# Strassen products of an MLP: operand sums made one product earlier, first summands written into accumulating banks

## The chip, the core and the metric

The kernel runs on one core of a Trainium2 chip. The time is the device time of one execution, in microseconds (us). Five engines work side by side, each with its own list of instructions: PE (TensorE, matmuls), ACT (ScalarE), DVE (VectorE), POOL (GpSimd) and SP (SyncE, which here issues all DMAs). They wait for each other by semaphores: `wait_ge(s, v)` holds an engine until the semaphore s has reached v.

## The reference

Batch 8, sequence 576, model width 512, all in fp32. An attention-like stage and a first mixing stage come first; the change is in the last stage:

```
def _moe2_ref(x, w_tok1, w_tok2, w_ch1, w_ch2):
    xt = x.transpose(0, 2, 1)
    h = np.maximum(xt @ w_tok1, 0.0) @ w_tok2
    u = x + h.transpose(0, 2, 1)
    h2 = np.maximum(u @ w_ch1, 0.0) @ w_ch2
    return (u + h2).astype(np.float32)
```

u has 8*576 = 4608 rows (tokens) of 512; `w_ch1` is 512 x 1536 and `w_ch2` is 1536 x 512. The output is [8, 576, 512].

## The kernel before, in words

Four phases follow each other: A (attention and first mixing), B (token mixing, which makes u), C (the **first product**, g = relu(u w_ch1)) and D (the **second product**, out = u + g w_ch2). Phases hand each other work at the seams through `nxt` and `prev`.

Each fp32 matmul is made of three: the operand is split into a rounded part `hi` (a copy to fp32r by ACT) and a rest `lo` (a subtraction by DVE), and `split_matmul` does hi*hi, hi*lo and lo*hi. C and D also use the Strassen-Winograd form: a 2x2 block product with seven block products (FIRST, SECOND, SHARED, MIDDLE, THIRD, LATE, LAST) in place of eight. The price is sums: four sums of the weight's blocks (made once), four sums of the moving operand's blocks per group, and seven sums of the results.

The tokens come in six **groups** of 768. C does 36 **units** (six groups of NI = 6 slices of w_ch1's columns); a unit is seven products of two depth tiles, 42 matmuls of 128x384. Its operand is `raw_u`, loaded once a group; `prep_hi` and `prep_lo` (L1222, L1226) split it, POOL makes its four sums (`prep_sum`). Results leave a bank by ACT copies (L1380, L1385, L1392) and DVE additions; a relu of all four blocks (L1366) ends the unit, and SP stores the blocks in `g_scratch` (L1316). Beside it, every second unit takes one of 14 steps that split `w_ch2` and its sums (ACT L1282, POOL L1292, stores L1273 and L1274).

D does six groups; a group is seven products for two column tiles j with six depth tiles, 252 matmuls of 128x384. SP loads the four blocks of g (`raw_g`, L1496). Two of the four operand sums are made by POOL (`first_sum`, `third_sum`: L1764, L1770), two by DVE (L1717, L1722). Each product needs a split: ACT L1528, DVE L1532. Its seven result sums, and the additions of u (`u2_left`), are shared by ACT, DVE and POOL (L1773, L1778); DVE transposes each result (L1679), and SP stores it in four DMAs of 48 KB (L1544). The seven split weights (`weights_down`, 1536 KB each) are read at the seam of C and D, as the memory of C's weights comes free.

The order of the work is written out by hand: each engine's list is the order of the calls in `scalar`, `vector`, `gpsimd`, `tensor` and `sync`. All DMAs go through SP's one queue.

## Time and profile before

| | us |
|---|---|
| median of 3 runs | 1306.64 (1303.24 to 1309.28) |
| the profiled execution, whole | 1305.25 |
| its span, first to last instruction | 1303.4 |
| phases A and B, until the last matmul before C | 0 to 708 |
| C, first product | 708 to 981 |
| D, second product | 981 to 1303.4 |

Busy shares of the span are 93% for PE, 60% DVE, 43% POOL, 39% ACT. A busy share averages phases with different limits, so the table is to be read by phase. PE's busy time contains the overlap of neighbouring matmuls: what counts for the time is the distance between their starts, and the idle time in front of them.

### The profile page before, as it was taken

How to read it: one execution, taken by the hardware profiler on the slowest of the kernel's cores; microseconds unless marked ns; L12 is line 12 of the kernel's file. 1: busy time of each engine (PE TensorE's matmuls, PEld its weight loads, DVE VectorE, ACT ScalarE, POOL GpSimd, SP SyncE). 2: the span in 40 equal slices, each digit the busy share in tenths (PEclk: the TensorE clock that was granted, in tenths of full speed). 3: DMA queues.
4: the chain of work that ended last, by engine and by line, in shares of the span. 5: the costliest groups of instructions: out<-in, count | busy, mean ns of one | idle time of the engine just before them, and what ended most of it. 6: DMA issues, size and time to landing. Idle time of an engine off the chain costs nothing.

```text
span 1303.4 us, 20411 instructions
## 1 busy us (share of the span) xinstructions
PE 1215.8 (93%) x7746; PEld 1175.6 (90%) x7746; DVE 787.4 (60%) x1120; ACT 503.3 (39%) x747; POOL 565.6 (43%) x331
## 2 busy tenths in 40 slices
PE   6899999999999999899999999999994599999998
PEld 5799999999999989799899899899994599899997
DVE  3866667665757666655455445444422688777865
ACT  3534333332424242423333455545541334324331
POOL 4443535253434444402631444544410574485473
PEclk9999999999999999999999999999997799999999
DMA  9921424242424200325464555555349276476462
GB/s 253 172 46 43 77 67 72 72 72 72 72 72 72 45 27 0 116 90 180 159 204 152 191 203 229 198 194 209 155 184 404 95 204 193 95 224 183 120 189 49
DMA packets 249438, 177.82 MB, mean 136 GB/s; under 512 B 196256, under 2 KB 221472, under 8 KB 247456
## 3 DMA queue, kind: packets, MB, share of 16 engines
q1 hardware_dynamic: 249376, 176.98, 46.3%
q8 instruction: 41, 0.67, 0.2%
q14 instruction: 21, 0.17, 0.0%
HBM read 109.31 MB, written 67.63 MB: 136 GB/s over the span
## 4 chain that ended last, share of the span: by engine, by line
PE 49%; issue 15%; DVE 13%; POOL 10%; DMA 6%; ACT 4%; SPq 3%; DVEq 0%; POOLq 0%; ACTq 0%
PE bank L42 13%; PE bank L43 12%; PE bank L44 12%; DVE z_g_split L1532 3%; PE bank L1163 2%; PE bank L1165 2%; PE bank L1164 2%; POOL tokens_raw_g L1764 2%; PE bank L236 2%; DMA u_raw_g<-g_scratch 2%; DVE weights_fraction L605 1%; PE bank L918 1%; POOL z_z L770 1%; POOL weights_down_t L1778 1%; DMA tokens_raw_g<-g_scratch 1%
## 5 line engine op out<-in xcount | busy, mean ns | idle before, releaser
L42 PE MATMUL bank<-weights_tok,z_z 128*128 128x288 f32 x576 | 175.1, 304 | 14.7 <-ACT z_z L455 9.3
L43 PE MATMUL bank<-weights_tok,z_z 128*128 128x288 f32 x576 | 171.0, 297 | 0.0
L44 PE MATMUL bank<-weights_tok,z_z 128*128 128x288 f32 x576 | 170.9, 297 | 0.0
L770 POOL TENSOR_TENSOR z_z<-tokens_cos,z_z 128x512 fp32r<-128x512 f32 x32 | 51.8, 1618 | 177.3 <-ACT z_z L455 176.4
L42 PEld LDWEIGHTS bank<-weights_tok,z_z 128*128 128x128 f32 x576 | 109.4, 190 | 18.2 <-ACT z_z L455 10.7
L755 POOL TENSOR_TENSOR weights_rms_inverse<-weights_mean_squares,weights_minus_half 128x8 f32<-128x8 f32 x40 | 65.6, 1640 | 137.7 <-DVE weights_mean_squares L572 137.5
L42 PE MATMUL bank<-z_g_split,weights_down 128*128 128x384 f32 x240 | 83.7, 349 | 36.8 <-DVE z_g_split L1532 36.8
L43 PEld LDWEIGHTS bank<-weights_tok,z_z 128*128 128x128 f32 x576 | 109.5, 190 | 0.0
L44 PEld LDWEIGHTS bank<-weights_tok,z_z 128*128 128x128 f32 x576 | 109.3, 190 | 0.0
L1532 DVE TENSOR_TENSOR z_g_split<-tokens_raw_g,z_g_split 128x2304 fp32r<-128x2304 f32 x16 | 65.2, 4074 | 45.0 <-ACT z_g_split L1528 45.0
L462 ACT ACTIVATE weights_x_channel_major<-u_u 128x288 fp32r<-128x288 f32 x64 | 28.4, 444 | 150.2 <-DVE u_u L633 150.2
L43 PE MATMUL bank<-z_g_split,weights_down 128*128 128x384 f32 x240 | 83.0, 346 | 0.0
L44 PE MATMUL bank<-z_g_split,weights_down 128*128 128x384 f32 x240 | 82.8, 345 | 0.0
L42 PEld LDWEIGHTS bank<-z_g_split,weights_down 128*128 128x128 f32 x240 | 47.2, 197 | 38.2 <-issue 38.2
L42 PE MATMUL bank<-weights_x_channel_major,weights_ch 128*128 128x288 f32 x256 | 77.5, 303 | 0.0
L43 PE MATMUL bank<-weights_x_channel_major,weights_ch 128*128 128x288 f32 x256 | 75.4, 294 | 0.0
L44 PE MATMUL bank<-weights_x_channel_major,weights_ch 128*128 128x288 f32 x256 | 75.4, 294 | 0.0
L1528 ACT ACTIVATE z_g_split<-tokens_raw_g 128x2304 fp32r<-128x2304 f32 x16 | 34.1, 2129 | 100.8 <-POOL tokens_raw_g L1764 43.2
L44 PE MATMUL bank<-z_u_slot,weights_up 128*128 128x384 f32 x216 | 72.2, 334 | 0.0
L42 PE MATMUL bank<-z_u_slot,weights_up 128*128 128x384 f32 x216 | 72.2, 334 | 0.0
L43 PE MATMUL bank<-z_u_slot,weights_up 128*128 128x384 f32 x216 | 72.1, 334 | 0.0
L631 DVE TENSOR_TENSOR u_u<-bank,weights_x_channel_major 128x288 f32<-128x288 f32 x64 | 29.1, 455 | 68.3 <-PE bank L44 67.6
(234 smaller groups left out, 3767.0 us busy)
## 6 DMA issues: line engine op xcount, KB each, us to landing
g_scratch<-attention_staged SPq DMA_DIRECT2D x36, 768.0 KB, 3.3
tokens_raw_g<-g_scratch SPq DMA_DIRECT2D x12, 1152.0 KB, 7.4
weights_down<-w_scratch SPq DMA_DIRECT2D x7, 1536.0 KB, 13.6
x_scratch<-u_u SPq DMA_DIRECT2D x8, 1152.0 KB, 4.2
u_scratch<-u_u SPq DMA_DIRECT2D x8, 1152.0 KB, 6.3
weights_raw_u<-u_scratch SPq DMA_DIRECT2D x6, 1536.0 KB, 9.1
qkv_u_left<-u_scratch SPq DMA_DIRECT2D x6, 1536.0 KB, 6.6
qkv_k<-in_k_dram SPq DMA_DIRECT2D x32, 256.0 KB, 4.7
```

The costliest lines, as they stand in the source:

```text
L42: eng.matmul(out, w[0], x[0], start=first, stop=False)
L43: eng.matmul(out, w[0], x[1], start=False, stop=False)
L44: return eng.matmul(out, w[1], x[0], start=False, stop=last)
L236: mm = pe.matmul(ps_out[j % 2][:, hp * P:(hp + 1) * P], qt[:, j % 2, hp, :], kvbd[:, hp, :], start=True, stop=True)
L462: act.activation(x_half(0, c, half), u[:, c, half * HALF:(half + 1) * HALF], ACT.Copy).then_inc(a_uhi, 1)
L631: dve.tensor_tensor(ug, ps_acc[g % 4][:, 0:HALF], x_half(0, c, half).bitcast(F32), ALU.add).then_inc(d_u1, 1)
L755: gp.tensor_tensor(rms_inv[:, i, :], msq[:, i, :], minus_half[:, :], ALU.pow).then_inc(g_pow, 1)
L770: gp.tensor_tensor(z[1][:, j, :], cos_t[:, j % 3, :], z[0][:, j, :].bitcast(F32), ALU.subtract).then_inc(g_zlo, 1)
L1163: eng.matmul(out, w[0], x[0], start=False, stop=False, skip_group_check=True)
L1164: eng.matmul(out, w[0], x[1], start=False, stop=False, skip_group_check=True)
L1528: act.activation(slot(g, k)[0][:, :, :], operand(g, k)[:, :, :], ACT.Copy).then_inc(a_hi, 1)
L1532: dve.tensor_tensor(slot(g, k)[1][:, :, :], operand(g, k)[:, :, :], slot(g, k)[0][:, :, :].bitcast(F32), ALU.subtract).then_inc(d_lo, 1)
```

## The change

**Operand sums.** C makes not only the four blocks of g but also the four sums that D needs, and stores seven blocks of 128x384 per unit (`g_scratch` grows from 4 to NP = 7 blocks). D loads seven ready operands a group into a ring of four buffers (`load_operand`), splits each and makes no sums. The order of the products is now FIRST, SHARED, MIDDLE, SECOND, THIRD, LATE, LAST.

**First summands.** Where a result was bank + tile in SBUF, the first summand is now written into the bank itself (ACT copies bank to bank, L1402 and L1418 of the new file; DVE adds into a bank) and the product accumulates onto it. Four short matmuls (`open_bank`) open these banks at C's start. In D, DVE writes u + summand into the bank.

**C's order.** Three of a unit's products (THIRD, LATE, LAST) run inside the next unit, between its own four. ACT does each block's relu on its own as it leaves the bank, DVE makes the sums t1 to t4 in `staged`. The store of unit n is issued two units later. Three of a group's splits (`PREP_OWN`) are made in the group's own first unit, four (`PREP_NEXT`) in units 2 to 5 of the group before; `raw_u` is loaded in unit 1 and not in unit 0.

**POOL.** It has nothing left in D, and in C no result sums.

**The seam.** D's weights 1 to 6 are read in two parts around the store of unit 34; the third operand waits for that store, the fourth for the last one. D's first product for j = 0 runs before C's last.

```diff
--- before.py
+++ after.py
...
-    PREP_LO = {(B - 3, 4): 0, (B - 3, 5): 1, (B - 2, 4): 2, (B - 1, 2): 3}
+    PREP_HI = {B - 3: [FIRST], B - 2: [SHARED], B - 1: [MIDDLE, SECOND]}
+    PREP_LO = {(B - 3, 4): FIRST, (B - 2, 4): SHARED, (B - 1, 2): MIDDLE, (B - 1, 4): SECOND}
...
+FIRST, SHARED, MIDDLE, SECOND, THIRD, LATE, LAST = range(NP)
...
+    def bank(i):
+        return banks[i][:, 0:CH]
+    def bank_a(n):
+        return bank(n % 2)
+    def bank_b(n):
+        return bank(2 + n % 2)
+    bank_c, bank_e, bank_f = bank(4), bank(5), bank(6)
...
-    PREP_LO = {(1, 1): [FIRST], (2, 1): [SECOND], (3, 1): [SHARED], (4, 1): [MIDDLE], (5, 0): [THIRD],
-               (5, 1): [LATE], (5, 2): [LAST]}
-    PREP_SUM = {1: [0], 2: [1], 3: [2], 4: [3]}
...
+    PREP_NEXT = {2: [FIRST], 3: [SHARED], 4: [MIDDLE], 5: [SECOND]}
+    PREP_OWN = [THIRD, LATE, LAST]
+    PREP_SUM = {2: [0], 3: [1, 2], 5: [3]}
...
+    def store(sp, n):
+        g, i = divmod(n, NI)
+        sp.wait_ge(d_t4, n + 1)
+        sp.dma_start(g_dram[g, :, i, :, :], staged[n % 2][:, :, :]).then_inc(s_g[n % 2], DMA)
...
-            if i == 0 and g + 1 < NG:
+            if i == 1 and g + 1 < NG:
                 load(sp, g + 1)
             if n == 2 * NP + 1:
                 w2_load(sp, 1)
...
-            sp.wait_ge(a_relu, n + 1)
-            sp.dma_start(g_dram[g, :, i, :, :], staged[n % 2][:, :, :]).then_inc(s_g[n % 2], DMA)
+            if n >= 2:
+                store(sp, n - 2)
             if n in W2_UNIT:
                 w2_store(sp, W2_UNIT[n])
...
+            if n == UNITS - NI + 2:
+                sp.wait_ge(p[LAST], n - 2)
...
                 nxt["load_first"](sp)
+        nxt["load_weights"](sp, range(1, 5))
+        store(sp, UNITS - 2)
+        nxt["load_weights"](sp, range(5, NP))
+        sp.wait_ge(s_g[0], DMA * UNITS // 2)
+        nxt["load_third"](sp)
+        store(sp, UNITS - 1)
...
+        def open_bank(out):
+            pe.matmul(out, wu[FIRST][0][:, 0, 0:P], slot(0, FIRST)[0][:, 0, :], start=True, stop=True)
...
+        for n in range(UNITS):
+            wait(pe, d_c22, n - 1)
+            wait(pe, a_f, n - 1)
+            if n == 0:
+                pe.wait_ge(a_hi, 1)
+                for b in (bank_b(0), bank_b(1), bank_c):
+                    open_bank(b)
+                pe.wait_ge(*prev["d_u"])
+                open_bank(bank_f)
+            product(n, FIRST, bank_a(n))
+            if n > 0:
+                third(n - 1)
+            wait(pe, a_t5, n)
+            product(n, SHARED, bank_e)
+            if n > 0:
+                late(n - 1)
+            pe.wait_ge(a_b, n + 1)
+            product(n, MIDDLE, bank_a(n), onto=True)
+            product(n, SECOND, bank_b(n), onto=True)
+            if n > 0:
+                last(n - 1)
+        third(UNITS - 1)
+        late(UNITS - 1)
+        nxt["first"](pe, 0, 0)
+        last(UNITS - 1)
...
+        def relu(n, k, src, ready, done):
+            act.wait_ge(*ready)
+            act.activation(staged[n % 2][:, k, :], src, ACT.Relu).then_inc(done, 1)
+        def relu21(n):
+            relu(n, SECOND, bank_f, (p[LAST], n + 1), a_g21)
+        for n in range(UNITS + 2):
+            if n >= 2:
+                relu21(n - 2)
+            if n < UNITS:
+                if n == 0:
+                    act.wait_ge(*prev["d_u"])
+                act.wait_ge(p[FIRST], n + 1)
+                act.activation(bank_b(n), bank_a(n), ACT.Copy).then_inc(a_b, 1)
+            if 1 <= n <= UNITS:
+                if n == 2:
+                    act.wait_ge(*prev["stored"])
+                wait(act, s_g[(n - 1) % 2], DMA * ((n - 1) // 2))
+                relu(n - 1, FIRST, bank_b(n - 1), (p[SECOND], n), a_g11)
+                relu(n - 1, LATE, bank_c, (p[THIRD], n), a_g12)
+            if n < UNITS:
+                act.wait_ge(p[SHARED], n + 1)
+                wait(act, d_c22, n - 1)
+                act.activation(t5[n % 2][:, :], bank_e, ACT.Copy).then_inc(a_t5, 1)
+            if n == UNITS:
+                nxt["hi"](act, 0, SHARED)
+            if 1 <= n <= UNITS:
+                act.wait_ge(p[LATE], n)
+                wait(act, a_g21, n - 1)
+                act.activation(bank_f, bank_a(n - 1), ACT.Copy).then_inc(a_f, 1)
+                relu(n - 1, THIRD, staged[(n - 1) % 2][:, THIRD, :], (d_c22, n), a_g22)
+            if n < UNITS:
+                g, i = divmod(n, NI)
+                if i == 0:
+                    for k in PREP_OWN:
+                        prep_hi(act, g, k)
+                elif g + 1 < NG:
+                    for k in PREP_NEXT.get(i, []):
+                        prep_hi(act, g + 1, k)
+                if n in W2_UNIT:
+                    w2_hi_step(act, W2_UNIT[n])
...
+        def t4(n):
+            st = staged[n % 2]
+            dve.wait_ge(a_g21, n + 1)
+            dve.wait_ge(d_t2, n + 1)
+            dve.tensor_tensor(st[:, LAST, :], st[:, SECOND, :], st[:, MIDDLE, :], ALU.subtract).then_inc(d_t4, 1)
+        def t1(n):
+            st = staged[n % 2]
+            dve.wait_ge(a_g11, n + 1)
+            dve.wait_ge(a_g12, n + 1)
+            dve.tensor_tensor(st[:, SHARED, :], st[:, LATE, :], st[:, FIRST, :], ALU.subtract).then_inc(d_t1, 1)
+        def c22(n):
+            dve.wait_ge(a_f, n + 1)
+            wait(dve, s_g[n % 2], DMA * (n // 2))
+            dve.tensor_tensor(staged[n % 2][:, THIRD, :], bank_a(n), t5[n % 2][:, :], ALU.add).then_inc(d_c22, 1)
+        def u4(n):
+            dve.wait_ge(p[MIDDLE], n + 1)
             dve.wait_ge(a_t5, n + 1)
...
+            wait(dve, a_g12, n)
+            dve.tensor_tensor(bank_c, bank_a(n), t5[n % 2][:, :], ALU.add).then_inc(d_u4, 1)
+        def t2_t3(n):
+            st = staged[n % 2]
+            dve.wait_ge(a_g22, n + 1)
+            dve.wait_ge(d_t1, n + 1)
+            dve.tensor_tensor(st[:, MIDDLE, :], st[:, THIRD, :], st[:, SHARED, :], ALU.subtract).then_inc(d_t2, 1)
+            dve.tensor_tensor(st[:, LATE, :], st[:, THIRD, :], st[:, LATE, :], ALU.subtract).then_inc(d_t3, 1)
+        for n in range(UNITS + 2):
+            if n >= 2:
+                t4(n - 2)
+            if 1 <= n <= UNITS:
+                t1(n - 1)
+                c22(n - 1)
+            if n < UNITS:
+                u4(n)
+            if 1 <= n <= UNITS:
+                t2_t3(n - 1)
+            if n < UNITS:
+                g, i = divmod(n, NI)
+                if i == 0:
+                    for k in PREP_OWN:
+                        prep_lo(dve, g, k)
+                elif g + 1 < NG:
+                    for k in PREP_NEXT.get(i, []):
+                        prep_lo(dve, g + 1, k)
...
+            if n == UNITS:
+                nxt["lo"](dve, 0, SHARED)
...
-            gp.tensor_tensor(staged[n % 2][:, 3, :], t3[n % 2][:, :], t5[n % 2][:, :], ALU.add).then_inc(g_c22, 1)
...
+    def load_operand(sp, M):
+        g, k = divmod(M, NP)
+        wait(sp, d_lo, M - NR + 1)
+        sp.dma_start(raw[M % NR][:, :, :], g_dram[g, :, :, k, :]).then_inc(s_q[M % NR], DMA)
...
+    def load_weights(sp, ks):
+        for k in ks:
+            sp.wait_ge(prev["p"][k - 1], UNITS)
+            load_weight(sp, k)
+    def load_third(sp):
+        load_operand(sp, 2)
+        sp.wait_ge(prev["d_c22"], UNITS)
+        load_u2(sp, 0)
...
+    STORES = {3: [0], 4: [1, 2], 5: [3], 6: [4, 5, 6]}
     def sync(sp):
-        load_quarter(sp, 0, 1)
-        load_u2(sp, 0)
-        for s in prev["stored"]:
-            sp.wait_ge(*s)
-        load_quarter(sp, 0, 3)
+        sp.wait_ge(*prev["stored"][1])
+        load_operand(sp, 3)
         for g in range(NG):
...
+            for k in range(NP):
+                M = NP * g + k
+                if g > 0 and k == 0:
+                    store(sp, g - 1, 7)
+                    load_u2(sp, g)
+                if M + NR < TOTAL:
+                    load_operand(sp, M + NR)
+                for o in STORES.get(k, []):
+                    store(sp, g, o)
...
+    def first(pe, g, j):
+        if g == 0 and j == 1:
+            pe.wait_ge(prev["d_c22"], UNITS - 1)
+            pe.wait_ge(prev["a_f"], UNITS - 1)
+        elif g > 0:
+            pe.wait_ge(d_e, NJ * (g - 1) + j + 1)
+            pe.wait_ge(d_c22, NJ * (g - 1) + j + 1)
+        product(pe, g, FIRST, j, bank_a[j])
...
+        for M in range(2, TOTAL):
+            hi(act, *divmod(M, NP))
...
+        def seed_b(g, j):
+            dve.wait_ge(p[FIRST], NJ * g + j + 1)
+            if j == 0:
+                dve.wait_ge(s_u, DMA * (g + 1))
+            if g == 0:
+                dve.wait_ge(prev["a_g11"], UNITS - 1 + j)
+            dve.tensor_tensor(bank_b[j], bank_a[j], residual(j, 0, 0), ALU.add).then_inc(d_b, 1)
+        def take_shared(g, j):
+            dve.wait_ge(p[SHARED], NJ * g + j + 1)
+            dve.tensor_tensor(t12[j][:, :], bank_e[j], residual(j, 0, 1), ALU.add).then_inc(d_t12, 1)
+            wait(dve, d_x, 8 * (g - 1) + 5 + j)
+            dve.tensor_tensor(t22[j][:, :], bank_e[j], residual(j, 1, 1), ALU.add).then_inc(d_t22, 1)
+        def seed_c(g, j):
+            dve.wait_ge(p[MIDDLE], NJ * g + j + 1)
+            dve.wait_ge(d_t12, NJ * g + j + 1)
+            if g == 0:
+                dve.wait_ge(prev["a_g12" if j == 0 else "a_g21"], UNITS)
+            dve.tensor_tensor(bank_c[j], bank_a[j], t12[j][:, :], ALU.add).then_inc(d_c, 1)
+        def seed_e(g, j):
+            dve.wait_ge(p[LATE], NJ * g + j + 1)
+            dve.tensor_tensor(bank_e[j], bank_a[j], residual(j, 1, 0), ALU.add).then_inc(d_e, 1)
+        def c22(g, j):
+            dve.wait_ge(d_t22, NJ * g + j + 1)
+            dve.tensor_tensor(t22[j][:, :], bank_a[j], t22[j][:, :], ALU.add).then_inc(d_c22, 1)
...
             if g > 0:
                 out21(g - 1, 1)
...
+            split(M + 2)
+            seed_b(g, 0)
+            seed_b(g, 1)
+            split(M + 3)
+            take_shared(g, 0)
+            take_shared(g, 1)
+            split(M + 4)
+            seed_c(g, 0)
+            seed_c(g, 1)
+            split(M + 5)
             out11(g, 0)
...
             out11(g, 1)
...
+            split(M + 6)
             out12(g, 0)
...
             out12(g, 1)
+            split(M + 7)
+            seed_e(g, 0)
+            c22(g, 0)
+            seed_e(g, 1)
+            c22(g, 1)
             out22(g, 0)
...
+            split(M + 8)
+            out22(g, 1)
             out21(g, 0)
...
         out21(NG - 1, 1)
...
-    g_dram = nc.dram_tensor("g_scratch", [GROUPS, P, FT, 4, CH], F32).ap()
+    g_dram = nc.dram_tensor("g_scratch", [GROUPS, P, FT, NP, CH], F32).ap()
...
```

In C, SP issues for one group's load of `raw_u` and what stands around it; `g_scratch` is the store of a unit, `w_scratch` the two halves of a step on w_ch2. Before:

```order
L1316 DMA g_scratch<-attention_staged 128x1536
L1213 DMA weights_raw_u<-u_scratch 128x4x768
L1316 DMA g_scratch<-attention_staged 128x1536
L1273 DMA w_scratch<-qkv_down_hi 128x768
L1274 DMA w_scratch<-qkv_down_lo 128x768
```

The same place after:

```order
L1269 DMA w_scratch<-qkv_down_hi 128x768
L1270 DMA w_scratch<-qkv_down_lo 128x768
L1210 DMA weights_raw_u<-u_scratch 128x4x768
L1303 DMA g_scratch<-attention_staged 128x2688 x2
L1269 DMA w_scratch<-qkv_down_hi 128x768
L1270 DMA w_scratch<-qkv_down_lo 128x768
```

The load now stands right behind the two stores of a step on w_ch2, and the unit's store, 2688 elements wide in place of 1536, right behind the load.

In C, ACT's instructions of one unit that also has a step on w_ch2 (L1282), before:

```order
L1392 ACTIVATE qkv_up_t_0_0<-bank 128x384
L1380 ACTIVATE u_up_t_1_0<-bank 128x384
L1366 ACTIVATE attention_staged<-attention_staged 128x1536
L1385 ACTIVATE u_up_t_1_0<-bank 128x384
L1222 ACTIVATE z_u_slot_0<-weights_raw_u 128x768
```

After, with relus at L1390, copies bank to bank at L1402 (for SECOND) and L1418 (for LAST), the t5 copy at L1412 and the step on w_ch2 at L1278:

```order
L1390 ACTIVATE attention_staged<-bank 128x384
L1402 ACTIVATE bank<-bank 128x384
L1390 ACTIVATE attention_staged<-bank 128x384 x2
L1412 ACTIVATE qkv_up_t_1_0<-bank 128x384
L1418 ACTIVATE bank<-bank 128x384
L1390 ACTIVATE attention_staged<-attention_staged 128x384
L1219 ACTIVATE tokens_u_slot_0<-weights_raw_u 128x768
L1278 ACTIVATE qkv_down_hi<-qkv_raw_down 128x768
```

Seven short instructions take the place of three copies and one long relu. The copy that LAST needs (L1418) now stands behind two relus (L1390 x2) that write into `staged`.

In D, DVE's instructions around the MIDDLE product of a group, before (L1532 split, L1717 operand sum, L1679 transpose):

```order
L1532 TENSOR_TENSOR qkv_g_split_1<-attention_raw_g_0,qkv_g_split_0 128x2304
L1717 TENSOR_TENSOR attention_raw_g_0<-tokens_raw_g_0,attention_raw_g_0 128x2304
L1679 STREAM_TRANSPOSE attention_x_out_0<-weights_down_t_1_0 128x384
L1532 TENSOR_TENSOR z_g_split_1<-attention_raw_g_0,z_g_split_0 128x2304
L1684 TENSOR_TENSOR weights_down_t_0_0<-bank,weights_down_t_0_0 128x384
```

After (L1581 split, L1682 first summand of C11, L1686 and L1688 additions of u, L1695 first summand of C12):

```order
L1581 TENSOR_TENSOR qkv_g_lo_0<-attention_raw_g_0,qkv_g_hi_0 128x2304
L1682 TENSOR_TENSOR bank<-bank,qkv_u_left 128x384 x2
L1581 TENSOR_TENSOR tokens_g_lo_0<-attention_raw_g_0,z_g_hi_0 128x2304
L1686 TENSOR_TENSOR weights_down_t_0_0<-bank,qkv_u_left 128x384
L1688 TENSOR_TENSOR weights_down_t_0_0<-bank,qkv_u_left 128x384
L1686 TENSOR_TENSOR weights_down_t_1_0<-bank,qkv_u_left 128x384
L1688 TENSOR_TENSOR weights_down_t_1_0<-bank,qkv_u_left 128x384
```

The two operand sums are gone from DVE, and the additions of u, which were POOL's, have come to it; L1682 reads `u2_left`.

## Rows read from the trace of the kernel before

**Rows 1.** By stretch: us, busy (count), PE clock, DMA share, GB/s; C, D.

```profile
708.00:981.00 273.00, 265.87 (x1514) 263.31 (x1512) 123.43 (x183) 139.88 (x194) 114.72 (x78) 0.99 0.53 198
981.00:1300.00 319.00, 271.89 (x1512) 268.40 (x1512) 219.57 (x151) 101.77 (x78) 167.42 (x73) 0.94 0.59 175
```

**Rows 2.** PE's waits in D: in total, times, longest.

```profile
PE bank L42 <- DVE z_g_split L1532: 36.8, 5, 15.1
```

**Rows 3.** Timeline of PE in D's first group: start, us, what [idle before].

```profile
982.20 0.41 PE L42 MATMUL bank<-qkv_g_split,weights_down 128*128 128x384 f32 x1 [1.23 <-DVE qkv_g_split L1532]
...
1027.47 0.66 PE L42 MATMUL bank<-z_g_split,weights_down 128*128 128x384 f32 x1 [14.62 <-DVE z_g_split L1532]
```

**Rows 4.** One later group of D, by stretch.

```profile
1084.30:1131.40 47.10, 43.90 (x252) 43.31 (x252) 35.67 (x25) 16.35 (x14) 28.13 (x12) 1.00 0.60 168
```

**Rows 5.** Timeline of PE around C's longest wait.

```profile
844.75 0.44 PE L1163 MATMUL bank<-z_u_slot,weights_up 128*128 128x384 f32 x1 [3.14 <-DVE u_up_u L1411]
...
846.28 0.52 PE L42 MATMUL bank<-tokens_u_slot,weights_up 128*128 128x384 f32 x1
...
849.73 0.33 PE L43 MATMUL bank<-z_u_slot,weights_up 128*128 128x384 f32 x1
```

**Rows 6.** The chain at C's start: start, us, what.

```profile
708.22 0.47 DVE u_u L1065
...
709.26 0.63 SPq L1268
...
712.67 2.51 SPq L1268
```

**Rows 7.** Groups by form in C: count, busy, mean ns, idle before.

```profile
L1222 ACT ACTIVATE z_u_slot<-weights_raw_u 128x768 fp32r<-128x768 f32 x21 | 17.3, 840 | 14.6 <-DMA weights_raw_u<-u_scratch 9.9 <-DVE u_u L1065 4.7
L1380 ACT ACTIVATE u_up_t<-bank 128x384 f32<-128x384 f32 x18 | 8.9, 492 | 27.1 <-PE bank L44 27.1
L1411 DVE TENSOR_TENSOR u_up_u<-bank,u_up_t 128x384 f32<-128x384 f32 x18 | 10.0, 554 | 19.8 <-PE bank L1165 19.8
L1292 POOL TENSOR_TENSOR qkv_down_lo<-qkv_raw_down,qkv_down_hi 128x768 fp32r<-128x768 f32 x14 | 25.9, 1847 | 0.0
```

**Rows 8.** Timeline of ACT, two splits back to back.

```profile
751.77 1.57 ACT L1222 ACTIVATE z_u_slot<-weights_raw_u 128x768 fp32r<-128x768 f32 x2
```

**Rows 9.** Groups by form in D.

```profile
L1528 ACT ACTIVATE z_g_split<-tokens_raw_g 128x2304 fp32r<-128x2304 f32 x16 | 34.1, 2129 | 100.8 <-POOL tokens_raw_g L1764 43.2 <-DMA tokens_raw_g<-g_scratch 29.4 <-DVE tokens_raw_g L1717 18.8
L1532 DVE TENSOR_TENSOR z_g_split<-tokens_raw_g,z_g_split 128x2304 fp32r<-128x2304 f32 x16 | 65.2, 4074 | 45.0 <-ACT z_g_split L1528 45.0
L1532 DVE TENSOR_TENSOR z_g_split<-u_raw_g,z_g_split 128x2304 fp32r<-128x2304 f32 x4 | 10.1, 2515 | 0.0
```

**Rows 10.** DMAs issued from 708 to 720: KB each, us to landing.

```profile
qkv_raw_down<-in_moe_w_ch_dram SPq DMA_DIRECT2D x4, 384.0 KB, 8.2
g_scratch<-attention_staged SPq DMA_DIRECT2D x1, 768.0 KB, 8.9
```

**Rows 11.** DMAs of one steady group of C.

```profile
g_scratch<-attention_staged SPq DMA_DIRECT2D x6, 768.0 KB, 3.3
weights_raw_u<-u_scratch SPq DMA_DIRECT2D x1, 1536.0 KB, 8.8
```

**Rows 12.** Transfers from 975 to 1015, the seam.

```profile
DMA packets 3392, 15.17 MB, mean 379 GB/s; under 512 B 175, under 2 KB 1865, under 8 KB 2623
```

**Rows 13.** Transfers of one later group of D.

```profile
q1 hardware_dynamic: 16464, 7.87, 60.0%
qkv_u_left<-u_scratch SPq DMA_DIRECT2D x1, 1536.0 KB, 6.6
```

**Rows 14.** Timeline at the end, DVE and SP.

```profile
1297.23 0.56 DVE L1699 TENSOR_TENSOR weights_down_t<-bank,weights_down_t 128x384 f32<-128x384 f32 x1 [1.49 <-PE bank L44]
1297.83 0.58 DVE L1679 STREAM_TRANSPOSE tokens_x_out<-weights_down_t 128x384 f32<-128x384 f32 x1
1289.58 2.00 SPq L1544 DMA_DIRECT2D out_dram<-attention_x_out  x4
```

508 lines of the change are left out of this document (130 added, 378 removed).

## The prediction, made before the changed kernel ran

> **What bounds the kernel now.** I read the split of the span into stretches first, then PE's waits, then PE's timeline at the seam of C and D, and last the durations and the DMAs. C and D issue 1512 matmuls each, C in 273 us and D in 319 us and its tail [rows 1]. One group of D is 252 matmuls; in a group in which PE idles 3.4 of 47.1 us they take 43.7 us, which is 0.173 us from start to start [rows 4]. So 1512 of them stream in 262.2 us. PE has no wait of its own making; everything above 262.2 is a wait for somebody else, and the change can only win there. What there is to win before:
>
> - C: 273.0 - 262.2 = 10.8 us. Half of it is one stop of 3.14 us, after which the granted clock halves for a while: matmuls of 0.52 us instead of 0.33 [rows 5]. About ten of them at twice the distance cost 1.5 us.
> - D up to its last matmul at 1297.2: 316.2 - 262.2 = 54.0 us. In the first group PE waits 1.2 and 14.6 us for splits [rows 3] and 15.1 us between them, its longest wait, and these are most of what it waits for in D [rows 2]. Behind either long wait the first matmul takes 0.66 us [rows 3] and half clock lasts longer than after the stop in C, which I put at 2.7 us each. That is 36.4. The other 17.6 lie in the later groups, 3.4 us in each of four (one row stands for them) [rows 4], and some 4 us in the rest of the first and the last.
> - The tail: DVE's last sum at 1297.2, its transpose, four output DMAs: 6.2 us [rows 14].
>
> Together 71.0 us.
>
> **D, later groups.** The change takes two operand sums from DVE and all work from POOL. DVE's split of 2304 columns takes 2.5 us where POOL is quiet and 4.07 on average in the form that meets POOL's sums [rows 9]. DVE's new list per group is seven splits (17.6 us), twelve additions at 0.55 [rows 7] (6.6) and eight transposes at 0.58 [rows 14], 4.6: 28.8 us of 43.7. ACT keeps seven splits at 2.13 (14.9) [rows 9]. A product takes 6.24 us; its hi can start when the product three before it is done, so hi and lo are ready 6.24 - 2.13 - 2.5 = 1.6 us and one whole product ahead of PE. The tightest place is the first summand of C11. DVE needs `u2_left` for it, SP may load that only after the last output of the group before, and MIDDLE needs the bank 12.5 us into the group. The last three outputs are ready from 0.9 us before the group's end on; their stores take SP 2.0 us each [rows 14], until 5.1 us into the next group; the load lands 6.6 us later [rows 13], at 11.7; with 0.55 for DVE that is 12.3. I take 0.4 us of waiting for each of five groups, 2.0 us in all.
> The transfers per group were 60% of 47.1 = 28.3 us [rows 13]. Three operands more of 1.18 MB at 379 GB/s [rows 12] make it 37.6, of 43.7.
>
> **C's start.** ACT and DVE split three operands less before C. The four bank openings and FIRST wait for DVE's last sum of B, which ends at 708.7 [rows 6]; before, PE went on at 708.0. +0.8 us.
>
> **C, compute.** ACT per unit: seven instructions of 0.49 and 1.6 of 0.84 [rows 7], 4.8 of 7.28 us. DVE: six of 0.55 and 1.17 splits of about 1.2, 4.7 us. An ACT copy from bank to bank and a DVE addition into a bank are not in the trace. The nearest rows are the same sizes into SBUF (0.49 and 0.55), which I take; nothing in them suggests a gain, at twice the price ACT has 5.8 us a unit, still under 7.28. In an undisturbed unit the copy for LAST ends at 4.9 us and PE wants it at 6.2. So compute costs nothing; PE's cover for LAST is 1.3 us.
>
> **C, the store.** That cover is what the new wait uses up. ACT's relu of unit n, made in unit n+1, overwrites the buffer of unit n-2, and the store of unit n-2 is issued two units late. ACT waits for it *in front of* the t5 copy and the copy for LAST. In unit 1 of a group four things meet. From the start of unit 0: LATE ends at 4.3, copy 4.9, C22 5.5, relu 6.0, three splits and the step on w_ch2 on ACT to 9.0 (0.73 apart) [rows 8], POOL's part 1.85 [rows 7] to 10.9. SP holds everything until then. At 3.7 us into unit 1 it issues the step's two stores (0.79 MB), then `raw_u` (1.57 MB), then the store of unit n-2 (1.38 MB). 3.74 MB at 379 GB/s [rows 12] are 9.9 us, and 1.2 us are not transfer (a store of 0.79 MB takes 3.3, of which 2.1 are) [rows 11]. The store is in at 14.8, and ACT wanted it at 9.1. Behind it ACT's three copies 0.38 apart end at 16.5, LAST was due at 13.5: 3.0 us of PE, and as after the stop of 3.14 us another 1.5 at half clock. That a small store waits behind loads issued before it is in the trace: 8.9 us for the first one of C, behind `w_ch2` and `raw_u`, against 3.3 in a steady group [rows 10, 11]. It happens in the four groups whose unit 0 has a step (units 7, 13, 19, 25): 18.0 us. In unit 15 the four loads of `w_ch2` stand in front of the store instead: SP issues them from 709.3 to 715.2 when they come first in C [rows 6] and they land after 8.2 [rows 10]. The store then comes some 4 us later than in the other four, 5.8 us of PE and 1.8 at half clock: 7.6 us. Sum for C 25.6 us, against 10.8 before. Bounds: none of it, if the store goes through quickly (at 417 GB/s, a tenth above a mean that contains gaps, and without half clock it is 2 us each, 8 in all; with LAST's cover at its best, nothing), to 40 us if a transfer behind a mixed queue takes half as long again.
> The Trainium skill, "DMA: Bandwidth & Descriptors", section "Queues, rings and completion order", says that each DMA engine takes one queue's descriptors in the order of the ring; by that the store can't overtake `raw_u`, and the trace's 8.9 us agree. Were they to share the engines evenly, the store would be in some 3 us sooner and C's waits would be 5 us or less.
>
> **The seam.** T is the start of unit 35. The products of that unit, THIRD and LATE among them, D's FIRST for both column tiles and C's LAST give PE work until T+16.6, SHARED until T+22.9. MIDDLE needs the third operand. SP's queue before it: store 33 (issued at T+4.1, since DVE makes D's first split before that unit's last sum), four weights, store 34, two weights, the operand: 13.4 MB, at 379 GB/s 35.4 us, landed at T+40.2. hi 2.13 and lo 2.5 make T+44.9, the first summand T+45.7. PE idles 22.8 us, then 2.7 at half clock. SECOND needs the fourth operand, which may be loaded when store 35 is in: u and the store take 4.1 and 3.6 us more, T+46.5, the load 6.6 (u's time, for a little more data) [rows 13], hi and lo 4.7: T+57.8, where PE is free at T+54.5: 3.3 us and 1.5 at half clock. Later operands come every 3 us and stay ahead. Sum 30.3 us, against 36.4 before. Bounds 24 and 36: the rate a tenth above or below.
> The Trainium skill, "SBUF — State Buffer", section "A bandwidth-pool intuition that's wrong (but worth ruling out)", gives about 358 GB/s between HBM and a core. That speaks against a change that moves 21 MB more out and 21 MB more in. Here 379 GB/s were the mean over 40 us, so the trace disagrees; by the page's figure the seam would cost 2 us more and the four units about 2 together.
>
> **The tail.** The last sum before the last transpose is gone: 6.2 - 0.6 = 5.6 us.
>
> **The sum.** After: 0.8 + 25.6 + 30.3 + 2.0 + 5.6 = 64.3 us, before 71.0: 6.7 us less. From the profiled execution's 1305.25 that gives 1298.6; the median of the runs stands 1.4 above it, so 1300.
>
> **Rivals.**
> *The store is in time.* C's 25.6 us fall to 5 or less, D as above: 1300 - 21 = 1279, down to 1272 if the seam also goes at its better bound. For it: the same queue carried raw_u in 8.8 us behind a store [rows 11] without a stop of PE, and the small store itself needs 3.3. Against it: the order of the queue, and ACT's place in it. Chance 0.27.
> *u comes late in D* (slower). Each group then waits for the first summand of C11, on which DVE's whole list stands. For it: after the change 37.6 of 43.7 us of the transfers are taken, and `raw_u`, of the same size, needs 8.8 us in company [rows 11] where u needed 6.6. It decides as soon as u lands later than 11.9 us into the group. At 3.7 us more in each of five groups, and after each such stop some slow matmuls: 5 * (3.3 + 0.4) = 18.5, 1318. Against it: no operand is queued ahead of it then, only output stores. Chance 0.20.
> *The seam doesn't shrink and the mixed queue is slower*: all transfers a tenth slower, stops in C of 4 us, seam 34: 1300 + 4 + 4 = 1308, no change to be measured. Chance 0.08.
> Left for the forecast: 0.45, own range 1289 to 1311.
>
> **Range and chances.** 0.5% of 1306.6 is 6.5 us, about what a measurement can tell, so the lines are 1300.1 and 1313.2. The forecast lies on the first: I give half of it to faster, 0.43 of it to same, the rest to slower. Faster 0.27 + 0.23 = 0.50; same 0.19 + 0.07 = 0.26; slower 0.24. Range 1273 to 1316.
>
> **What would show it.** In the changed trace: ACT waits for `g_scratch` stores in units 8, 14, 16, 20 and 26 of C, and PE for the copy at L1418 right after, about 3 us each; if C runs near 265 us, the first rival holds. D's later groups 43.7 to 44.3 us long, POOL empty; groups of 47 with DVE waiting for `u2_left` would be the second. One idle stretch of 23 us at D's MIDDLE and one of 4 at SECOND; if the first is 15 or less, the seam was overpriced. A DVE instruction into a bank above 0.8 us, or ACT above 7 us a unit, would break the compute part.

## The result, and the profile after

The changed kernel takes 1328.07 us (median of 4 runs, 1324.23 to 1331.25), the kernel before 1306.01: ratio 1.0167, 95% interval 1.0123 to 1.021. Slower by 1.7%; 1300 was forecast, with a range to 1316. The profiled execution took 1324.95, its span is 1323.1, 19.7 us more than before. The times leave out slow executions; there was one, of experiment 1, with 2004 us at a mean granted clock of 0.555.

PE still gives the measure. From C's first matmul to the 1512th after it, and from there to the end of the last one, I subtract the 262.2 us in which 1512 of them stream. In the kernels with the change the four bank openings count among C's 1512, so four of C's matmuls (0.7 us) stand under D. The same for the kernel before:

| waits and slow matmuls, us | before | forecast | after |
|---|---|---|---|
| C's start | 0 | 0.8 | -0.9 |
| C | 12.0 | 25.6 | 44.9 |
| D's first group (seam) | 35.5 | 30.3 | 29.0 |
| D's other five groups | 17.3 | 2.0 | 12.4 |
| tail | 6.2 | 5.6 | 5.2 |
| sum | 71.0 | 64.3 | 90.6 |

The change does win 11 us in D and 1 in the tail. It loses 33 in C. The start of C is no result: in the eleven traces of kernels with the change, whose code is the same up to there, it lies between 706.8 and 712.3 us. The two stretches of the changed kernel, to set beside [rows 1] (us, busy of PE, its weight loads, DVE, ACT, POOL with counts, granted PE clock, DMA share, GB/s):

```profile
707.00:1014.00 307.00, 278.18 (x1514) 274.49 (x1513) 179.32 (x251) 153.09 (x301) 87.72 (x43) 0.94 0.64 243
1014.00:1318.00 304.00, 271.06 (x1519) 268.12 (x1517) 165.64 (x166) 89.14 (x46) 0.00 (x0) 0.96 0.83 255
```

C is 34 us longer, its clock fell from 0.99 to 0.94 and the transfer rate rose from 198 to 243 GB/s; in D POOL is empty. What PE waits for in C and D, in total, times, longest; before, in D, it was a split [rows 2]:

```profile
PE bank L1158 <- DVE bank L1682: 29.0, 6, 20.3
PE bank L1158 <- ACT bank L1418: 27.9, 8, 5.0
PE bank L1158 <- issue: 3.4, 1, 3.4
```

L1418 is ACT's copy for LAST in C, L1682 the first summand that DVE writes for C11 in D. Both were named in the forecast. So read the five long stops of C, at one of them. SP's list, with the w_ch2 step's two stores (the second is left out), then raw_u, then the store of unit 5 and, in the same row, that of unit 6 (start, duration of the issue):

```profile
760.41 0.32 SPq L1269 DMA_DIRECT2D w_scratch<-qkv_down_hi  x1
...
761.25 0.58 SPq L1210 DMA_DIRECT2D weights_raw_u<-u_scratch  x1
761.88 3.95 SPq L1303 DMA_DIRECT2D g_scratch<-attention_staged  x2
```

ACT's list: its relu of unit 7 needs the buffer of unit 5 and waits 7.92 us for that store; the copy for LAST stands behind it:

```profile
764.84 0.47 ACT L1402 ACTIVATE bank<-bank 128x384 f32<-128x384 f32 x1 [0.51 <-PE bank L44]
773.23 0.87 ACT L1390 ACTIVATE attention_staged<-bank 128x384 f32<-128x384 f32 x2 [7.92 <-DMA g_scratch<-attention_staged]
774.35 0.51 ACT L1418 ACTIVATE bank<-bank 128x384 f32<-128x384 f32 x1
```

And PE, which needs the copy, with its first slow matmul:

```profile
774.92 0.69 PE L1158 MATMUL bank<-z_u_slot,weights_up 128*128 128x384 f32 x1 [4.92 <-ACT bank L1418]
775.40 0.52 PE L1159 MATMUL bank<-z_u_slot,weights_up 128*128 128x384 f32 x1
```

The store landed at 773.2, 12.8 us after SP issued the first of the four transfers. PE wanted the copy at 770.0. The bracket is the idle time; measured from start to start, as the table does and as stops are given from here on, a stop is 0.17 us longer. Such stops of 4.8 to 5.2 us stand in just the five places forecast (774.9, 826.4, 848.7, 885.0 and 937.8). Behind each the granted clock drops to half for a while (0.50 is 1.2 GHz, 1.00 is 2.4):

```profile
775.00:781.00 6.00, 6.00 (x19) 6.00 (x20) 3.33 (x6) 3.24 (x6) 2.98 (x2) 0.50 0.04 18
```

The distances between starts sum to 1.7 to 2.9 us more than at full clock, per stop.

What none of my terms had is a sixth stop, in unit 34, near C's end (two of about 1 us, in units 24 and 28, were not in them either):

```profile
1001.76 0.45 PE L1158 MATMUL bank<-z_u_slot,weights_up 128*128 128x384 f32 x1 [2.69 <-ACT bank L1418]
```

At the seam, PE waits for the first summand on which MIDDLE rests, and then in front of SECOND, against the 15.1 and 14.6 us of before [rows 2, 3]:

```profile
1048.67 0.69 PE L1158 MATMUL bank<-z_g_hi,weights_down 128*128 128x384 f32 x1 [20.33 <-DVE bank L1682]
...
1061.14 0.66 PE L1158 MATMUL bank<-qkv_g_hi,weights_down 128*128 128x384 f32 x1 [3.44 <-issue]
```

The profile names no releaser for the second. DVE's row shows it: the split of the fourth operand, which SECOND reads, ends at 1061.04.

```profile
1058.48 2.56 DVE L1581 TENSOR_TENSOR qkv_g_lo<-attention_raw_g,qkv_g_hi 128x2304 fp32r<-128x2304 f32 x1 [9.40 <-ACT qkv_g_hi L1574]
```

SP's list there: four weights, store 34, two weights, then nothing until store 34 is in, 20 us later:

```profile
1008.32 3.45 SPq L1541 DMA_DIRECT2D weights_down<-w_scratch  x4
1013.11 0.32 SPq L1303 DMA_DIRECT2D g_scratch<-attention_staged  x1
1013.48 0.93 SPq L1541 DMA_DIRECT2D weights_down<-w_scratch  x2
1032.92 0.53 SPq L1538 DMA_DIRECT2D attention_raw_g<-g_scratch  x1
```

In each later group of D DVE waits for u_left. SP issues it behind the stores of the last outputs of the group before, 6.5 us into the group:

```profile
1187.88 0.52 SPq L1546 DMA_DIRECT2D qkv_u_left<-u_scratch  x1
```

DVE's list, with its first addition that needs it:

```profile
1194.77 1.03 DVE L1682 TENSOR_TENSOR bank<-bank,qkv_u_left 128x384 f32<-128x384 f32 x2 [8.39 <-DMA qkv_u_left<-u_scratch]
```

And PE's, with the product behind that:

```profile
1195.39 0.44 PE L1158 MATMUL bank<-z_g_hi,weights_down 128*128 128x384 f32 x1 [1.35 <-DVE bank L1682]
```

It lands 6.9 us after its issue, and PE is idle for 1.35 us; in the five groups the stops are 1.5 to 2.4. Before, a whole group lost 3.4 [rows 4]. The new instructions cost what their neighbours cost: a copy from bank to bank 0.486 us, where I took 0.49 (count, busy, mean ns, idle before).

```profile
L1418 ACT ACTIVATE bank<-bank 128x384 f32<-128x384 f32 x35 | 17.0, 486 | 12.7 <-PE bank L1160 12.7
```

### The profile page after: what moved, and what is told of

Read it like the earlier page. It is cut to its first block, busy times and chain, and to the rows that moved or that the text cites. A ratio compares the mean times of both kernels' runs of the same rounds, so it can differ in the third digit from the quotient of the medians.

```text
span 1323.1 us, 20482 instructions
## 1 busy us (share of the span) xinstructions
PE 1226.0 (93%) x7750; PEld 1185.1 (90%) x7750; DVE 788.0 (60%) x1204; ACT 502.0 (38%) x819; POOL 369.2 (28%) x223
## 4 chain that ended last, share of the span: by engine, by line
PE 49%; DMA 13%; issue 13%; DVE 8%; POOL 6%; ACT 5%; SPq 5%; DVEq 0%; POOLq 0%; ACTq 0%
DMA g_scratch<-attention_staged 10%; PE bank L42 9%; PE bank L44 9%; PE bank L43 9%; PE bank L1158 6%; PE bank L1160 6%; PE bank L1159 6%; SPq L1593 3%; DMA qkv_u_left<-u_scratch 3%; PE bank L236 2%; POOL qkv_down_lo L1288 1%; DVE weights_fraction L605 1%; POOL z_z L770 1%; PE bank L918 1%; DVE tokens_cos L602 1%
## 5 line engine op out<-in xcount | busy, mean ns | idle before, releaser
L42 PE MATMUL bank<-weights_tok,z_z 128*128 128x288 f32 x576 | 175.1, 304 | 14.6 <-ACT z_z L455 9.2
L1158 PE MATMUL bank<-z_g_hi,weights_down 128*128 128x384 f32 x240 | 82.5, 344 | 25.4 <-DVE bank L1682 25.4
L1444 DVE TENSOR_TENSOR attention_staged<-attention_staged 128x384 f32<-128x384 f32 x36 | 30.8, 855 | 94.1 <-ACT attention_staged L1390 94.0
L462 ACT ACTIVATE weights_x_channel_major<-attention_u 128x288 fp32r<-128x288 f32 x64 | 28.4, 444 | 150.4 <-DVE attention_u L633 150.4
L1390 ACT ACTIVATE attention_staged<-bank 128x384 f32<-128x384 f32 x108 | 50.4, 486 | 84.9 <-DMA g_scratch<-attention_staged 61.3
L1160 PE MATMUL bank<-z_g_hi,weights_down 128*128 128x384 f32 x240 | 81.7, 341 | 0.0
L1158 PE MATMUL bank<-z_u_slot,weights_up 128*128 128x384 f32 x192 | 66.6, 347 | 13.3 <-ACT bank L1418 13.3
L1158 PEld LDWEIGHTS bank<-z_g_hi,weights_down 128*128 128x128 f32 x240 | 46.3, 193 | 26.7 <-DVE bank L1682 26.7
L631 DVE TENSOR_TENSOR attention_u<-bank,weights_x_channel_major 128x288 f32<-128x288 f32 x64 | 29.1, 455 | 68.6 <-PE bank L44 68.3
L1159 PE MATMUL bank<-z_u_slot,weights_up 128*128 128x384 f32 x192 | 66.0, 344 | 0.0
L1160 PE MATMUL bank<-z_u_slot,weights_up 128*128 128x384 f32 x192 | 65.9, 343 | 0.0
L1158 PE MATMUL bank<-tokens_u_slot,weights_up 128*128 128x384 f32 x132 | 46.3, 350 | 15.5 <-ACT bank L1418 14.7
```

Source lines behind the costliest of these rows:

```text
L42: eng.matmul(out, w[0], x[0], start=first, stop=False)
L631: dve.tensor_tensor(ug, ps_acc[g % 4][:, 0:HALF], x_half(0, c, half).bitcast(F32), ALU.add).then_inc(d_u1, 1)
L1158: eng.matmul(out, w[0], x[0], start=False, stop=False, skip_group_check=True)
L1159: eng.matmul(out, w[0], x[1], start=False, stop=False, skip_group_check=True)
L1160: return eng.matmul(out, w[1], x[0], start=False, stop=last, skip_group_check=True)
L1390: act.activation(staged[n % 2][:, k, :], src, ACT.Relu).then_inc(done, 1)
```

## The experiments

The order is that of the questions: is it the place in the queue (1 and 2, and then raw_u in front), the size of packets or of the store, and then D, the seam, C's end, and what all of it is worth. "C" below is always the figure of the table's second row, from each kernel's own trace, and it is free of where C starts. Each ratio is taken to executions of the kernel before made beside that run (medians 1303.9 to 1304.3).

**1. Store ahead of raw_u.**

```diff
+            if n >= 2:
+                store(sp, n - 2)
             if i == 1 and g + 1 < NG:
                 load(sp, g + 1)
             if n == 2 * NP + 1:
                 w2_load(sp, 1)
-            if n >= 2:
-                store(sp, n - 2)
```

> The changed kernel with one change of SP's order in C: in unit n the store of unit n-2 is issued ahead of the load of raw_u (and, in unit 15, ahead of the four loads of w_ch2), not behind it. Theory (the store's place in the queue makes the five long stops): in units 7, 13, 19 and 25 the store no longer stands behind raw_u's 1.57 MB, only behind the two w_ch2 stores; it is issued at the same time and lands near 767.5 where it landed at 773.2, ACT wanted it at 765.3, and LAST has 1.3 us of cover: stops of 0 to 1 us in place of 4.9 and 2.9 at half clock, and the stop of unit 15/16 goes with them. Five times some 7 us: 1328 - 33 = 1295, at worst 1302. Rival 1 (ACT's and DVE's longer lists, or banks read and written by two engines, make the stops): the order of the queue changes nothing, 1328. Rival 2 (the queue is simply full): raw_u comes later and its split stops PE instead, 1320 or more.

1316.42 us, ratio to the kernel before 1.0096 (1.0066 to 1.0126). C starts at 712.3 in this trace and at 707.1 in that of the changed kernel, so its times are to be read 5.2 us earlier, and the time wins less than C does. The five stops near 5 us are gone and C fell from 44.9 to 30.2. The theory holds for them, but it gave 33 us and got 15. What is left stands in other units, among it four stops of 2.8 to 3.0 us, and begins as rival 2 said, with raw_u coming later. ACT's list, in unit 8 (two rows) and in unit 10:

```profile
773.23 0.87 ACT L1390 ACTIVATE attention_staged<-bank 128x384 f32<-128x384 f32 x2 [2.77 <-DMA g_scratch<-attention_staged]
...
778.09 0.85 ACT L1219 ACTIVATE tokens_u_slot<-weights_raw_u 128x768 fp32r<-128x768 f32 x1 [2.08 <-DMA weights_raw_u<-u_scratch]
...
792.38 0.87 ACT L1390 ACTIVATE attention_staged<-bank 128x384 f32<-128x384 f32 x2 [5.49 <-DMA g_scratch<-attention_staged]
```

raw_u is late now (778.09, 2.08 us). POOL's sum of it starts at 780.01, and its part of the w_ch2 step behind that:

```profile
780.01 1.84 POOL L1230 TENSOR_TENSOR weights_raw_u<-weights_raw_u 128x768 f32<-128x768 f32 x1 [12.38 <-DVE tokens_u_slot L1223]
781.81 2.15 POOL L1288 TENSOR_TENSOR qkv_down_lo<-qkv_raw_down,qkv_down_hi 128x768 fp32r<-128x768 f32 x1
```

SP holds the next store behind the step's stores (its issue, 784.82), and ACT waits for that one 5.49 us:

```profile
784.82 5.45 SPq L1303 DMA_DIRECT2D g_scratch<-attention_staged  x2
```

**2. The w_ch2 stores one unit later as well.**

```diff
             if n >= 2:
                 store(sp, n - 2)
+            if n - 1 in W2_UNIT:
+                w2_store(sp, W2_UNIT[n - 1])
             if i == 1 and g + 1 < NG:
                 load(sp, g + 1)
...
-            if n in W2_UNIT:
-                w2_store(sp, W2_UNIT[n])
```

> As e1, and the two w_ch2 stores of a step are issued one unit later too, behind the store of unit n-2, so that SP doesn't hold that store until POOL has finished the step. Theory: the store of unit 5 is issued when its last sum is made, at 757.5 in place of 761.9, with nothing ahead of it, and lands near 761.5, 4 us before ACT wants it. All stops of the first 30 units go, those of units 24 and 28 (1.0 and 1.1 us) perhaps too; the stop of 2.9 and 1.7 at half clock in unit 34, behind the first two operands and the first weight of D, stays: C 267 to 270 us in place of 306.9, in all 1290 to 1293, 3 us better than e1. Rival 1: 1328. Rival 2: the steps on w_ch2 are now late, and ACT, which waits for their stores in front of its own copies, stops PE in the even units: 1300 or more.

1300.03 us, 0.9976 (0.9957 to 0.9995), C 16.2. Taking SP out of POOL's hands was worth 14 us more. 7 to 10 us are missing against the forecast. ACT waits 0.18 us for the store now, and 3.77 for raw_u, which stands behind the stores:

```profile
766.24 0.88 ACT L1390 ACTIVATE attention_staged<-bank 128x384 f32<-128x384 f32 x2 [0.18 <-DMA g_scratch<-attention_staged]
...
774.10 0.85 ACT L1219 ACTIVATE tokens_u_slot<-weights_raw_u 128x768 fp32r<-128x768 f32 x1 [3.77 <-DMA weights_raw_u<-u_scratch]
```

**3. raw_u ahead of the w_ch2 stores.** The two calls of experiment 2 in the other order.

> As the kernel that stored first and put the w_ch2 stores one unit later, with raw_u's load ahead of those two stores. There C took 278.2 us: in units 8 and 20 ACT waited 3.8 us for raw_u (landed at 774.1) in front of the w_ch2 step, and everything behind it, POOL's sum, the step, SP, the next store, came late in turn. Theory (each of these stops is the lateness of whatever is queued last): raw_u lands 2.4 us sooner, at about 771.7, ACT wanted it at 770.3: the stops of 1.4 and 0.7 at half clock in four units fall below 0.5 each; C 271 to 273, in all 1293 to 1296. Rival: the lists of ACT, DVE and POOL in the even units are too long whatever comes when (ACT's next copies end after PE wants them): C stays at 278, 1300.

1300.78 us, 0.998 (0.9966 to 0.9993): no difference to be measured, though C is 14.0 in place of 16.2. C moved the right way by a third of what I expected, and the time is the rival's 1300; in four places a pair of short stops remains, 1.6 to 1.8 us a pair. What holds ACT and DVE there was not followed.

**4. Is raw_u slow because of its packets?** The store landed 1.7 us later than my 379 GB/s gave. In a stretch of raw_u (763 to 768), and in one of the stores behind it (769 to 773), the changed kernel moved:

```profile
DMA packets 455, 1.35 MB, mean 271 GB/s; under 512 B 16, under 2 KB 16, under 8 KB 454
```

```profile
DMA packets 197, 1.74 MB, mean 436 GB/s; under 512 B 24, under 2 KB 24, under 8 KB 39
```

The experiment reads raw_u of groups 1 to 5 from other places, in one run of 12 KB for each partition. The values are other ones, so only its times are of use; group 0, cut from the lines shown, is read as before.

```diff
-        sp.dma_start(raw[:, :, :], u2_dram[:, :, g * 2 * CH:(g + 1) * 2 * CH]).then_inc(s_u, DMA)
...
+        sp.wait_ge(*prev["stored"])
+        flat = u2_dram.rearrange("p c t -> p (c t)")
+        sp.dma_start(raw[:, :, :].rearrange("p c t -> p (c t)"),
+                     flat[:, g * NC * 2 * CH:(g + 1) * NC * 2 * CH]).then_inc(s_u, DMA)
```

> The changed kernel, but the raw_u of groups 1 to 5 is read from other places of u_scratch, so that each partition's part is one run of 12 KB (four runs of 3 KB before): the same 1.57 MB, other values. The question is why the stops took 4.9 us and not 3.0: of the 12.8 us from the step's first store to the landing of the g store, some 5.6 went to raw_u, at 288 GB/s, while the g store itself ran at 436. Theory packets: raw_u is slow because its packets are 3072 bytes where the g store's are 10752; in 12 KB packets it takes 3.6 us, the g store lands 2 us sooner, each of the four stops in units 7, 13, 19, 25 is 2.9 us with less half clock: 4 * 2 to 4 * 3 less, 1316 to 1320. Rival neighbours: raw_u is slow there because of what runs beside it (the store just before it, POOL's and ACT's work), since u_left in D has the same 3072-byte packets and ran at 400 GB/s; then raw_u still takes 5 us or more, the stops stay at 4.9, 1328.

1327.77 us, 1.0188 (1.0159 to 1.0217), C 42.1, stops of 4.7 to 5.5. With 12 KB packets raw_u moved hardly faster, at 305 GB/s:

```profile
DMA packets 147, 1.52 MB, mean 305 GB/s; under 512 B 16, under 2 KB 16, under 8 KB 25
```

So it is mostly not the packets. u_left, with packets of 3 KB, ran at 373 GB/s in D (1190 to 1193). And raw_u itself, with the same packets, ran faster in C where it stood right behind a g store and not behind the w_ch2 stores: in the kernel before (762 to 766), and in experiment 3 (767 to 772):

```profile
DMA packets 494, 1.50 MB, mean 376 GB/s; under 512 B 9, under 2 KB 9, under 8 KB 493
```

```profile
DMA packets 580, 1.73 MB, mean 345 GB/s; under 512 B 20, under 2 KB 20, under 8 KB 579
```

That speaks for the neighbours. But both kernels differ in more than that, so what slows raw_u is not shown.

**5. Do the added bytes make the stops?** The kernel stores only four of the seven blocks, and D reads one of these four in place of each of the others; the output is another.

```diff
-        sp.dma_start(g_dram[g, :, i, :, :], staged[n % 2][:, :, :]).then_inc(s_g[n % 2], DMA)
+        sp.dma_start(g_dram[g, :, i, 0:4, :], staged[n % 2][:, 0:4, :]).then_inc(s_g[n % 2], DMA)
...
-        sp.dma_start(raw[M % NR][:, :, :], g_dram[g, :, :, k, :]).then_inc(s_q[M % NR], DMA)
+        sp.dma_start(raw[M % NR][:, :, :], g_dram[g, :, :, k % 4, :]).then_inc(s_q[M % NR], DMA)
```

> The changed kernel, but each store of g takes four of the seven blocks (0.79 MB as before the change, in place of 1.38), and D loads blocks 0 to 3 in place of 4 to 6, so the loads keep their size; the waits and the order of every list are those of the changed kernel, the output is other. Theory (the stops come from the order: a small transfer waits behind 2.4 MB that are not urgent, and ACT waits for it ahead of its copies): a store of 0.59 MB less at 436 GB/s lands 1.4 us sooner, so the five long stops are 3.5 us and not 4.9, a little less at half clock with each, the one in unit 34 is 1.5 and not 2.9: C 296 us in place of 307, in all 1315 to 1319. Rival (the added bytes are the cost): without them the stops go altogether, as in the kernel before, C 270 or less, in all below 1295.

1316.7 us, 1.0096 (1.0059 to 1.0134), C 30.9, and five stops of 3.4 to 3.8 us:

```profile
PE bank L1158 <- ACT bank L1418: 17.2, 5, 3.7
```

The time is the theory's; the rival, with stops gone and a time below 1295, is out. The smaller store is worth 14 of the 33 us that C lost, and the order alone, at full size, 31 (C 14.0 in experiment 3). The two overlap, so they can't be added: the added bytes make the stops longer, and with the lists in order C is, bytes and all, 2 us above the kernel before. The sixth stop, in unit 34, went altogether, where I had said 1.5 us. The first group of D fell too, from 29.0 to 25.5.

**6. u_left early in D.**

```diff
                 if g > 0 and k == 0:
                     store(sp, g - 1, 7)
-                    load_u2(sp, g)
                 if M + NR < TOTAL:
                     load_operand(sp, M + NR)
+                if k == NP - 1 and g + 1 < NG:
+                    load_u2(sp, g + 1)
                 for o in STORES.get(k, []):
```

> The changed kernel with one change of SP's order in D: the load of u_left for group g+1 is issued before the stores of outputs 4 to 7 of group g, as soon as DVE has read the old u for the last time, not behind output 7. Theory (u comes late): the five stops of 1.5 to 2.4 us at C11's first summand go, D's groups take 43.7 to 44.0 us in place of 45.3 to 47.8: 9 to 11 us less, 1317 to 1319. Rival: the operand loads are what DVE really waits for, or the delayed output stores hold the transposes: groups of 45 and more, 1325 to 1328.

1315.19 us, 1.0086 (1.0059 to 1.0112). PE's waits in the last five groups, of the changed kernel and then of this one:

```profile
PE bank L1158 <- DVE bank L1682: 8.6, 5, 2.2
```

```profile
PE bank L1158 <- DVE bank L1696: 0.4, 1, 0.4
```

The five groups lose 1.4 us together and not 12.4. The theory holds, with its number.

**7. The seam in another order.**

```diff
-        nxt["load_weights"](sp, range(1, 5))
+        nxt["load_weights"](sp, range(1, 3))
         store(sp, UNITS - 2)
-        nxt["load_weights"](sp, range(5, NP))
+        store(sp, UNITS - 1)
         sp.wait_ge(s_g[0], DMA * UNITS // 2)
         nxt["load_third"](sp)
-        store(sp, UNITS - 1)
...
     def load_third(sp):
         load_operand(sp, 2)
+        sp.wait_ge(*prev["stored"][1])
+        load_operand(sp, 3)
         sp.wait_ge(prev["d_c22"], UNITS)
         load_u2(sp, 0)
+        load_weights(sp, [3])
...
     def sync(sp):
-        sp.wait_ge(*prev["stored"][1])
-        load_operand(sp, 3)
...
                     load_operand(sp, M + NR)
+                if M < 3:
+                    load_weights(sp, [M + 4])
```

> The changed kernel, C as it is, with another order of SP's list at the seam of C and D. Now: four weights (1 to 4), store 34, two weights, the third operand when store 34 is in, u_left, store 35, the fourth operand when that is in. Here: weights 1 and 2, store 34, store 35, third operand, fourth operand, u_left, weight 3, then operand 5, weight 4, operand 6, weight 5, operand 7, weight 6. Theory (MIDDLE waits only because 6.3 MB that nobody needs yet stand ahead of what it needs): u_left is in near 1039.5 on the profile's scale and MIDDLE starts at 1040 in place of 1048.7; SECOND, which waited for the fourth operand (3.4 us), follows at once: 12 us less, 1314 to 1318. Rival 1: the weights then come late, THIRD and LATE stop for them for 3 us or more each: 1322. Rival 2: the seam is bound by the sum of all bytes, not by their order: 1326 to 1328.

1326.57 us, 1.0172 (1.015 to 1.0193), which is the time of rival 2: half of the expected gain at the place, and next to none in the time. The first group loses 23.1 us in place of 29.0:

```profile
1042.95 0.69 PE L1158 MATMUL bank<-z_g_hi,weights_down 128*128 128x384 f32 x1 [13.35 <-DVE bank L1684]
...
1075.10 0.45 PE L1158 MATMUL bank<-qkv_g_hi,weights_down 128*128 128x384 f32 x1 [4.40 <-DVE bank L1701]
```

MIDDLE waits 13.35 us and not 20.33, SECOND no longer waits, but LAST does, 4.4 us: DVE's addition for it (L1701) stands behind the split of the next group's first operand, which is late. And of MIDDLE's wait the last part is no longer the operand's: DVE had split that at 1039.3 and then waited for u_left, which the new order puts behind the fourth operand:

```profile
1042.33 1.03 DVE L1684 TENSOR_TENSOR bank<-bank,qkv_u_left 128x384 f32<-128x384 f32 x2 [3.01 <-DMA qkv_u_left<-u_scratch]
```

So rival 2, the sum of the bytes, is not shown by this time. In the trace the other five groups take the gain back: they lose 20.2 us, against 12.4 in that of the changed kernel. 1.7 of it is a longer stop in the group right behind the seam (3.8 us for 2.1), which may be the seam's own lateness. For the rest their code differs in nothing, and they vary from trace to trace: 12.2 and 12.1 us in experiments 1 and 2, 17.1 in 3, 20.9 in 8. Behind a stop of some 2.2 us matmuls are slow for 1.6 us in some groups and for 0.1 in others. The changed kernel's own four runs show it too: 1324.2 and 1325.0 at a mean granted clock of 0.975 and 0.973, 1331.2 and 1331.3 at 0.970.

**8. D's first loads in three units.**

```diff
             if n == UNITS - NI + 2:
                 sp.wait_ge(p[LAST], n - 2)
                 sp.wait_ge(s_w2, 4 * DMA * NP)
-                nxt["load_first"](sp)
+            if n >= UNITS - NI + 2 and n < UNITS - NI + 5:
+                nxt["load_first"](sp, n - (UNITS - NI + 2))
```

(`load_first` issues the first operand, then the second, then the first weight, one at each call.)

> The changed kernel with one change: D's first two operands and its first weight (3.9 MB), which SP issues together in unit 32 of C behind store 30, are issued in units 32, 33 and 34, each behind that unit's store. Theory (the stop of 2.9 us and 1.7 at half clock in unit 34, which no one had priced, is store 31 behind 3.9 MB): it goes, C is 302.4 in place of 306.9, the seam stays at 29, in all 1323 to 1324. Rival: the same bytes only move the stop one or two units on, or to D's first products (the first weight comes later): 1328.

1323.97 us (1318.43 to 1331.16), 1.0137 (1.0115 to 1.0158). The median is the forecast, the spread is wider than the effect; the trace decides. The stop of unit 34 is gone, C is 40.1 and not 44.9, the seam 29.6.

**9. All of it.** Experiments 3, 6, 7 and 8 together, and raw_u's splits one unit later:

```diff
-    PREP_NEXT = {2: [FIRST], 3: [SHARED], 4: [MIDDLE], 5: [SECOND]}
+    PREP_NEXT = {3: [FIRST], 4: [SHARED], 5: [MIDDLE, SECOND]}
-    PREP_SUM = {2: [0], 3: [1, 2], 5: [3]}
+    PREP_SUM = {3: [0], 4: [1, 2], 5: [3]}
```

> All reorderings together, nothing of the change undone: in C store, raw_u, w_ch2 stores one unit later; raw_u's splits and POOL's sums one unit later (units 3 to 5 of a group in place of 2 to 5); D's first two operands and first weight issued in three units (32, 33, 34) in place of one; the seam in the order of the seam kernel; u_left early. Theory: C 264 to 268 (no stop at unit 34, 4.5 us less, none in the even units), seam 12 us less, D's later groups 43.7: 1306.6 - 13 - 9 + ... = counted from the changed kernel's 1328: C -39 to -42, seam -12, D -10: 1264 to 1268, 3% below the kernel before. Rival: the gains don't add, since a store or an operand that is early in one place takes the queue from another; then the stop at unit 34 or at MIDDLE comes back: 1275 or more.

1274.52 us, 0.9778 (0.9758 to 0.9798), 54 us below the changed kernel by the medians and 49 by the profiled executions. C loses 9.1 us, the first group 24.1, the other five 2.4:

```profile
PE bank L1158 <- DVE bank L1687: 12.5, 1, 12.5
PE bank L1158 <- DVE bank L1704: 5.2, 1, 5.2
PE bank L1158 <- ACT bank L1418: 3.0, 4, 0.8
PE bank L1158 <- ACT bank L1402: 1.8, 1, 1.8
```

7 to 11 us of the forecast are missing, and the time is half a microsecond from the rival's 1275. The seam won 5 us of the expected 12, with MIDDLE still waiting 12.5 and LAST 5.2, C 36 of 39 to 42, the later groups their 10. What the later splits are worth by themselves was not measured.

**10. The seam once more.** SP: weight 1, store 34, weight 2, third operand, store 35, u_left, fourth operand, weight 3; in D's first group DVE:

```diff
-            split(M + 7)
+            if g > 0:
+                split(M + 7)
             seed_e(g, 0)
             c22(g, 0)
             seed_e(g, 1)
             c22(g, 1)
+            if g == 0:
+                split(M + 7)
```

> The kernel with all reorderings (1274.5), with two more. At the seam SP issues weight 1, store 34, weight 2, third operand, store 35, u_left, fourth operand, weight 3, and so on: of what MIDDLE needs nothing stands behind store 35 but u_left. And in D's first group DVE makes the first summands of C21 and C22 ahead of the split of the next group's first operand, which came late there and held LAST for 5.2 us. Theory (each wait is for what stands ahead in a list): MIDDLE starts 4 to 6 us sooner, SECOND then waits for the fourth operand 1 to 3 us, LAST's 5.2 us go: 1265 to 1269. Rival: from 974 to 1030 the queue is full without a gap, so whatever is first, the bytes bound the seam; what MIDDLE and LAST win comes back at SECOND, THIRD and at the next group's FIRST: 1272 to 1275.

1275.87 us, 0.977 (0.9752 to 0.9788): the same as experiment 9. The first group loses 17.5 us and not 24.1, with MIDDLE at 9.2 and LAST at 2.7,

```profile
1004.65 0.69 PE L1158 MATMUL bank<-z_g_hi,weights_down 128*128 128x384 f32 x1 [9.19 <-DVE bank L1688]
...
1035.05 0.44 PE L1158 MATMUL bank<-qkv_g_hi,weights_down 128*128 128x384 f32 x1 [2.72 <-DVE bank L1705]
```

but the other five lose 8.1 in place of 2.4, 3.7 of it as stops in the next group. Of the 6.6 us won, 5.7 come back in D, and the time is a microsecond above the rival's 1272 to 1275, far from the theory's 1265 to 1269. Its reason, the sum of the bytes, is not shown: DVE still waits 2.5 us for u_left ahead of MIDDLE, so the list has an order left to try.

**11. The kernel before, with its seam in order.**

```diff
             if n == UNITS - 1:
-                nxt["load_weights"](sp)
+                nxt["load_weights"](sp, 2)
...
     def sync(sp):
         load_quarter(sp, 0, 1)
-        load_u2(sp, 0)
         for s in prev["stored"]:
             sp.wait_ge(*s)
         load_quarter(sp, 0, 3)
+        load_weight_(sp, 3)
+        load_u2(sp, 0)
+        for k in range(4, NP):
+            load_weight_(sp, k)
```

(`load_weights(sp, 2)` issues weights 1 and 2 and the third block.)

> The kernel before, with none of the change, and the same care at its seam: weights 1 and 2, third block of g, store 35, second block, fourth block, weight 3, u_left, weights 4 to 6; there all six weights stood ahead of store 35 and the last two blocks. It asks what the reorderings are worth without the change. Theory (the change pays once its transfers are in order, since it takes the 3.4 us from each later group of D and the sums from POOL): here only the seam's waits of 36 us shrink, by 10 to 17, as the fourth block comes 4 weights sooner: 1288 to 1295, so 15 to 20 us stay between it and the kernel with the change and all reorderings. Rival (all the gain is the order's): 1280 or less. A third way: POOL's and DVE's sums of the seam, not the loads, hold it: 1300 to 1306.

1287.61 us, 0.9876 (0.9857 to 0.9894), at the theory's lower end. The seam's 35.5 us become 17.4, with none of the change; its two waits of 15.1 and 14.6 us [rows 2, 3] are now:

```profile
996.87 0.66 PE L42 MATMUL bank<-z_g_split,weights_down 128*128 128x384 f32 x1 [8.53 <-DVE z_g_split L1536]
...
1009.90 0.66 PE L42 MATMUL bank<-z_g_split,weights_down 128*128 128x384 f32 x1 [3.93 <-DVE z_g_split L1536]
```

16 of the 29 us between experiment 9 and the kernel before are thus to be had by the order alone; 12 to 13 us stay for the changed kernel with everything in order, where I had said 15 to 20. That counts against a kernel before in which only the seam was put in order: its lists in C, where it loses 12.0 us, were left as they were, and what they would give is untested. By phases: C 9.1 against 12.0, first group 24.1 against 17.4, the others 2.4 against 16.4.

## Why the prediction was wrong

The forecast had 64.3 us of waits, the trace has 90.6; the difference of 26.3 is the miss (1324.95 in place of 1298.6). 11.3 of it are the size of C's store term, 8.0 are stops in C that had no term, 10.4 are D's later groups; the seam, C's start and the tail give 3.4 back. Step by step:

- *C, the store*, is the step that failed, and by its size. The mechanism was right in each part: units, queue order, ACT's place, PE's cover. That a DMA engine takes one queue's descriptors in ring order (the Trainium skill, "DMA: Bandwidth & Descriptors", "Queues, rings and completion order") carried it; experiments 1 and 2 agree, since with the store in front ACT's wait of 7.92 us fell to 2.77 and 0.18. Its price was 25.6 us and is 36.9: five stops of 25.0 together in place of 17.8, 11.9 of slow matmuls in place of 7.8. (The fifth, behind the loads of `w_ch2`, which I had at 5.8 us against 3.0 for the others, was as long as they were.) Two numbers did it. I priced 3.74 MB of mixed transfers at 379 GB/s, the mean over 40 us of the seam [rows 12]; here it was 292 (3.74 MB in 12.8 us), and raw_u itself 271. Its 8.8 us in company [rows 11] were in the same list of rows, and I used them only for the rivals. Why raw_u is slower here stays open (experiment 4). And I took the half clock behind a stop from the one stop of C before, 1.5 us [rows 5], and behind stops of 4.9 it is 1.7 to 2.9.
- *Not priced*: the stop of unit 34 (4.6 us), those of units 24 and 28 (2.9), and some 0.6 in small pieces. I had followed the store of unit n-2 behind raw_u and behind w_ch2, but not behind the 3.9 MB of D's first loads, which SP issues in the same place. Experiments 5 and 8, with smaller stores and with these loads spread, show the stop of unit 34 to be of the same mechanism: it goes in both. The stop in unit 24 is a wait for a split by DVE (0.8 us idle), and why that is late was not followed.
- *D, later groups*, 12.4 us and not 2.0. u_left was issued 6.5 us into the group, where I had 5.1 (output stores of 2.3 us and more each, not of 2.0 [rows 14]), and landed at 13.4 where I had 11.7. This is the slower rival's mechanism, at 10.4 us more than my 2.0 where the rival had 18.5. Experiment 6 shows it to be the whole of it.
- *The seam* was right: 29.0 for 30.3, with MIDDLE's 20.3 for 22.8 and SECOND's 3.4 for 3.3. *Compute and the tail* were right; the additions into banks and the copies between them cost what I took. Two of DVE's sums between tiles in SBUF did not: 1.07 and 0.86 us in the mean (L1438, L1444) and not 0.55, so that DVE works 5.0 us of a unit, not 4.7, still well under 7.28. *C's start* came out 1.7 us better than forecast, and that is luck: over the traces it varies by 5 us.

The range ended at 1316, about C's upper bound (40 us) set on the forecast and nothing else. C went past that bound, with 44.9, by the stops that had no term. And the range left out that C's and D's terms can be at their worst together, since both hang on one queue; by the same reason 0.24 for slower was too little.

The figure of 358 GB/s between HBM and a core (the Trainium skill, "SBUF — State Buffer", "A bandwidth-pool intuition that's wrong (but worth ruling out)") is passed here in stretches: 436 GB/s for the stores between 769 and 773. What hurt in C was first of all which transfer came first: the order gave 31 of its 33 us back with every byte kept. At the seam order counts as well (29.0 us became 24.1 and 17.5 in experiments 9 and 10, and 35.5 became 17.4 in the kernel before), and so do bytes (25.5 with the smaller stores of experiment 5); which of the two bounds it in the end is not shown.

## What to carry to other kernels

When an engine waits for a buffer to be stored, look at what else its list holds behind that wait, and at what the DMA queue holds ahead of that store: both lists must put the urgent first. A change that only moves work is measured fairly when the lists around it are put in order too; here the same change is 1.7% slower or 2.2% faster than the kernel before, and the kernel before was itself 1.2% slower than with its seam in order. And price a transfer by the row of its own kind and company, not by the best stretch of the queue.

## What the hardware showed

A load of 1.57 MB moved at 271 GB/s in C in packets of 3 KB, and at 305 in packets of 12 KB, where it followed two stores of w_ch2; the same load in packets of 3 KB moved at 376 and 345 where it followed a g store, a load with such packets at 373 in D, and the stores behind it, in packets of 10.5 KB, at 436. Behind a stop of PE of 4.9 us the matmuls at 1.2 GHz cost 1.7 to 2.9 us more. Stops of 2.1 to 3.0 us cost 0.1 or 1.6 to 2.0, and the length doesn't decide it: in D of the changed kernel one of 2.4 us cost 1.7, and in C of experiment 1 one of 3.0 us cost 0.1.
